# Strassen's seven half-size products for gate and value of the first MoE stage, on chunks of 512 tokens

## What is computed

```python
def _attn_ref(q, k, v, g_norm):            # 4 batches, 8 heads, 576 tokens, head size 64
    kv = np.einsum('bhsd,bhse->bhde', k, v)
    out = np.einsum('bhsd,bhde->bhse', q, kv)
    rms = np.sqrt(np.mean(out * out, axis=-1, keepdims=True) + 1e-06)
    return out / rms * g_norm
def _moe_ref(x, w_gate, w_val, w_out):     # 512 -> 1536 -> 512
    g = x @ w_gate
    silu = g * (1.0 / (1.0 + np.exp(-g)))
    return silu * (x @ w_val) @ w_out
def _moe2_ref(x, w_in, w_out):             # 512 -> 2048 -> 512
    h = x @ w_in
    return (np.maximum(h, 0.0) + np.log1p(np.exp(-np.abs(h)))) @ w_out
```

## Time and profile before

| | us |
|---|---|
| median of 3 runs | 936.55 (936.08 to 937.48) |
| profiled execution | 937.88 |
| its span | 936.03 |
| last product of the first stage issued, from the span's start | 514.2 |
| TensorE busy in the span | 906.2 |
| VectorE busy | 540.1 |
| ScalarE busy | 342.0 |
| GpSimd busy | 91.1 |

### The profile page before, as it was taken

How to read it: one execution, slowest core, us unless ns; L and a number is a source line. 1 busy time by engine, 2 the same in 40 slices (tenths; PEclk the granted TensorE clock), 3 DMA queues, 4 the chain that set the end, 5 groups by cost and what they waited for, 6 DMA issues and landing times.

```text
span 936.0 us, 13451 instructions
## 1 busy us (share of the span) xinstructions
PE 906.2 (97%) x5128; PEld 856.7 (92%) x5128; DVE 540.1 (58%) x1006; ACT 342.0 (37%) x597; POOL 91.1 (10%) x43
## 2 busy tenths in 40 slices
PE   6899899999999999999999699999999999999998
PEld 5789899999999999999999589999998999999997
DVE  3643344453444224224344997887877878878875
ACT  1435413232241001000222344545545554554543
POOL 2424400000000000000243900000000000000000
PEclk9999999999999999999999799999999999999999
DMA  9954461153111000000022300000000000000000
GB/s 251 164 155 125 134 133 26 42 114 73 44 45 56 1 1 1 0 0 0 26 88 91 113 1 1 34 0 0 34 0 0 34 0 0 34 0 0 34 1 34
DMA packets 84189, 44.18 MB, mean 47 GB/s; under 512 B 40768, under 2 KB 76736, under 8 KB 84160
## 3 DMA queue, kind: packets, MB, share of 16 engines
q1 hardware_dynamic: 84000, 43.80, 18.0%
q10 hardware_dynamic: 160, 0.00, 0.0%
HBM read 35.52 MB, written 8.26 MB: 47 GB/s over the span
## 4 chain that ended last, share of the span: by engine, by line
PE 87%; DVE 4%; DMA 3%; SPq 2%; ACT 2%; issue 1%; POOL 0%; DVEq 0%
PE bank L534 21%; PE bank L535 21%; PE bank L536 21%; PE bank L589 7%; PE bank L590 7%; PE bank L588 7%; DMA stage<-in_moe_w_out 2%; PE bank L460 2%; PE bank L475 1%; DMA v_rest<-in_v 1%; SPq L305 1%; ACT arena L664 1%; DVE x_lo L850 1%; DVE g_hi L872 0%; ACT L651 0%
## 5 line engine op out<-in xcount | busy, mean ns | idle before, releaser
L534 PE MATMUL bank<-x_hi,arena 128*128 128x384 f32 x960 | 324.8, 338 | 9.0 <-DVE x_lo L850 5.5
L536 PE MATMUL bank<-x_hi,arena 128*128 128x384 f32 x960 | 323.0, 336 | 0.0
L535 PE MATMUL bank<-x_lo,arena 128*128 128x384 f32 x960 | 322.6, 336 | 0.0
L534 PEld LDWEIGHTS bank<-x_hi,arena 128*128 128x128 f32 x960 | 180.9, 188 | 16.1 <-DVE x_lo L850 6.6
L535 PEld LDWEIGHTS bank<-x_lo,arena 128*128 128x128 f32 x960 | 181.0, 189 | 3.8
L536 PEld LDWEIGHTS bank<-x_hi,arena 128*128 128x128 f32 x960 | 181.1, 189 | 0.0
L881 DVE TENSOR_TENSOR act_a<-act_a,bank 128x384 f32<-128x384 f32 x72 | 39.8, 553 | 228.2 <-PE bank L536 227.0
L686 ACT ACTIVATE act_a<-bank 128x384 f32<-128x384 f32 x72 | 35.4, 492 | 289.6 <-PE bank L536 289.6
L422 POOL TENSOR_TENSOR arena<-stage,arena 128x1024 fp32r<-128x1024 f32 (+1 forms) x28 | 80.8, 2886 | 432.0 <-ACT arena L671 380.7
L707 ACT ACTIVATE act_a<-bank 128x384 f32<-128x384 f32 x96 | 47.3, 493 | 192.2 <-PE bank L536 192.2
L590 PE MATMUL bank<-arena,g_lo 128*128 128x512 f32 x288 | 113.8, 395 | 0.0
(11 more groups left out here) (55 smaller groups left out, 807.4 us busy)
## 6 DMA issues: line engine op xcount, KB each, us to landing
stage<-in_moe_w_out SPq DMA_DIRECT2D x28, 256.0 KB, 4.2
out_dram<-out_stage SPq DMA_DIRECT2D x18, 256.0 KB, 2.1
...
```

The costliest lines, as they stand in the source:

```text
L534: nc.tensor.matmul(ps, hi, rhs_hi, start=first, stop=False)
L535: nc.tensor.matmul(ps, hi, rhs_lo, start=False, stop=False)
L536: return nc.tensor.matmul(ps, lo, rhs_hi, start=False, stop=last)
```

## The change

**Seven products.** The four products of gate and value with two halves of the contraction (256 features each) and two halves of a chunk (256 tokens each) form a 2x2 by 2x2 block product. It is done with Strassen's seven products in Winograd's form instead of eight. A chunk has now `CH1` = 512 tokens; there are `NC1` = 4 such chunks, so `SEVEN` = 48 steps, and 12 further steps (`up_plain`) for the last 256 tokens, with gate and value as before. One product is 2 tiles of the contraction by 3 passes, 6 matmuls of 256 columns; `up_seven` has 7 of them, which go round banks 0 to 3 (`ps_of`). `down1` has 12 matmuls of 512 columns.

**Sums after the products.** VectorE adds up the banks: two additions in `add_early`, five in `add_late`, each of 256 columns with one input in a bank and one in SBUF; ScalarE copies the first product to `p1`. Gate and value stand in `s_buf` and `val`, one buffer each; silu, the product with the value, the rounding (now on ScalarE, `hi_g`) and the low part (`lo_g`) are done there for 512 columns.

**Sums ahead of the products, of the weights.** The split weights no longer fit. `raw1` keeps all 12 raw slices, loaded once, and each step splits them anew for the step after next: four sums of 256 columns on VectorE (`weight_sums`, into the one buffer `s_sum`), the rounding on ScalarE (`hi_raw` 768 columns, `hi_s` 1024, `hi_down` 512), the low parts on GpSimd (`lo_raw` 768, `lo_s` 1024, `lo_down` 512), into `w_up` and `w_down`, two buffers each.

**Of x.** For each chunk four sums of 512 columns on GpSimd (`x_sums`, at step 10), seven operands rounded on ScalarE (`hi_x`), and 14 low parts of 256 columns on VectorE (`lo_x`, at step 11). `s_buf` has only one buffer, so `add_early` waits for `lo_g` of the step before (`g_split`).

**Attention.** k'v runs in steps 0 and 1, tiles at `TILE_AT` = (2, 4, 6, 7, 9), both behind `down1` and in the bank of the seventh product. ScalarE copies a tile to SBUF first (`keep_o`) and squares it there; `normalize_kept` multiplies in SBUF. VectorE and ScalarE do a tile's work in the step after it.

**Second stage.** The same work. The first 8 slices of its weights are split by ScalarE and VectorE (`split_low2`) in the 12 plain steps, the last 8 by GpSimd alone after the last product of the first stage. `split_x` of its first chunk stands three steps ahead of the end of the first stage.

```diff
 def _(pool):
+        def lo_raw(k):
+            pool.wait_ge(hi_raw_ready, k)
...
+            nc.gpsimd.tensor_tensor(w_up[k % 2][:, 1, 0:size], src, w_up[k % 2][:, 0, 0:size].bitcast(F32),
+                                    ALU.subtract).then_inc(w_raw_ready, 1)
...
+        for k in range(STEPS1):
+            if k:
+                lo_down(k)
+            if k % NF1 == NF1 - 2 and k // NF1 + 1 < NC1:
+                x_sums(k // NF1 + 1)
+            if k + 2 < STEPS1:
+                lo_raw(k + 2)
+            if k + 2 < SEVEN:
+                lo_s(k + 2)
...
 def _(pe):
+            for t in range(2):
+                a, b = slice(op * QUAD + t * P, op * QUAD + (t + 1) * P), slice(t * HALF, (t + 1) * HALF)
+                last = passes(ps_of(k, x)[:, 0:HALF], w[:, 0, a], w[:, 1, a], xc[:, slot, 0, b], xc[:, slot, 1, b],
+                              t == 0, t == 1)
+            last.then_inc(prod_done, 1)
...
+            product(k, S3, 3)
+            pe.wait_ge(p1_kept, k + 1)
+            product(k, A22, 4)
+            pe.wait_ge(c11_ready, k + 1)
+            product(k, S1, 5)
+            pe.wait_ge(u2_ready, k + 1)
+            product(k, S4, 6)
...
+        for k in range(1, SEVEN):
+            up_seven(k)
+            down1(k - 1)
+            if k // NF1 < NATT:
+                attention_slot(k // NF1, k % NF1)
...
 def _(act):
+            keep_p1(k)
+            if tile:
+                square_kept(c + 1, TILE_AT.index(f - 1))
+            if k:
+                hi_down(k)
...
+            hi_raw(k + 2)
+            silu(k)
...
+            if k + 2 < SEVEN:
+                hi_s(k + 2)
+            hi_g(k)
...
 def _(dve):
+        def weight_sums(k):
...
+            dve.wait_ge(w_s_ready, k)
+            n = 4 * (k - 1)
+            nc.vector.tensor_tensor(s_sum[:, 0, :], a21, a22, ALU.add).then_inc(s_ready, 1)
+            nc.vector.tensor_tensor(s_sum[:, 2, :], a11, a21, ALU.subtract).then_inc(s_ready, 1)
+            dve.wait_ge(s_ready, n + 2)
+            nc.vector.tensor_tensor(s_sum[:, 1, :], s_sum[:, 0, :], a11, ALU.subtract).then_inc(s_ready, 1)
+            dve.wait_ge(s_ready, n + 3)
+            nc.vector.tensor_tensor(s_sum[:, 3, :], a12, s_sum[:, 1, :], ALU.subtract).then_inc(s_ready, 1)
...
+            dve.wait_ge(g_split, k)
+            dve.wait_ge(p1_kept, k + 1)
+            dve.wait_ge(prod_done, done_before(k) + 2)
+            nc.vector.tensor_tensor(s_buf[:, 0:HALF], p1[:, :], ps_of(k, 1)[:, 0:HALF], ALU.add).then_inc(c11_ready, 1)
...
+            add_late(k)
...
+                weight_sums(k + 2)
+            glu(k)
```

More of the change, by code:

```diff
@@ L40 @@
 ROWS = [P] * J + [REST]
+BLK = 32
+BB = S // BLK
+NA = P // BLK
+NATT = B - 1
+HALF = 256
+CH1 = 2 * HALF
+NC1 = TOKENS // CH1
+CB1, HB = CH1 // BLK, HALF // BLK
+SEVEN = NC1 * NF1
+STEPS1 = SEVEN + NF1
+OPS = 7
+A11, A12, A22, S1, S2, S3, S4 = range(7)
+XSLOTS = 10
+QUAD = 2 * P
+RAW1 = 4 * QUAD + DM
+UP1 = OPS * QUAD
+KV_AT = (0, 1)
+TILE_AT = (2, 4, 6, 7, 9)
+X_NEEDED = [4, NT + 4, 2 * NT + 3, 3 * NT + 3, 4 * NT]
 CH = 384
@@ L558, in down1 @@
+        def down1(k):
+            c, f = divmod(k, NF1)
+            n = width(k)
+            pe.wait_ge(w_down_ready, k + 1)
+            pe.wait_ge(g_split, k + 1)
             if f == 0:
                 pe.wait_ge(acc_free, c + 1)
+            w = w_down[k % 2]
             for t in range(KT):
[L561 to L562 removed]
+                a = slice(t * P, (t + 1) * P)
+                last = passes(acc_ps[t][:, 0:n], w[:, 0, a], w[:, 1, a], g_hi[k % 2][:, 0:n], g_lo[k % 2][:, 0:n],
+                              f == 0, f == NF1 - 1)
@@ new lines, in _ @@
+        store_x(NT - 2, xt_ps0[(NT - 2) % 2])
+        for j in range(1, 4):
+            hi_x(0, j)
+        hi_raw(1)
+        for j in range(4, OPS):
+            hi_x(0, j)
+        hi_s(1)
+        keep_p1(0)
+        store_x(NT - 1, xt_ps0[(NT - 1) % 2])
+        hi_raw(2)
+        silu(0)
+        hi_s(2)
+        hi_g(0)
+        for k in range(1, SEVEN):
+            step(k)
+        for k in range(SEVEN, STEPS1):
+            f = k - SEVEN
+            if f == 1:
+                store_y(NC1 - 1)
+            hi_down(k)
+            silu_plain(k)
+            if k + 2 < STEPS1:
+                hi_raw(k + 2)
+            hi_g(k)
+            for n in range(DVE_LOW2):
+                if step_under(n) + 1 == k:
+                    split_high2(n)
@@ L829, in normalize, with lo_x @@
                                     ALU.mult).then_inc(xn_ready, 1)
-        def split_x(n, chunk, used=None, count=0, tiles=range(KT), scaled=True):
-            for t in tiles:
+        def lo_x(c, j):
+            dve.wait_ge(xc_hi_ready, OPS * c + j + 1)
+            for t in range(2):
+                last = nc.vector.scalar_tensor_tensor(
+                    xc_part(c, j, 1)[:, :, t, :], x_operand(c, j)[:, :, t, :], gain[:, 0:1],
+                    xc_part(c, j, 0)[:, :, t, :].bitcast(F32), ALU.mult, ALU.subtract)
+            last.then_inc(xc_ready, 1)
@@ L836, in split_x @@
+        def split_x(n, chunk, used=None, count=0):
+            for t in range(KT):
                 if used is not None and t < KT - 1:
@@ new lines, in _ @@
+        dve.wait_ge(t_ready, 1)
+        nc.vector.tensor_tensor(x_sum(0, 1), x_block(0, 1, 1), x_sum(0, 0), ALU.subtract).then_inc(t_ready, 1)
+        dve.wait_ge(t_ready, 2)
+        nc.vector.tensor_tensor(x_block(0, 0, 1), x_block(0, 1, 1), x_block(0, 0, 1), ALU.subtract).then_inc(t_ready, 1)
+        lo_x(0, 1)
+        nc.vector.tensor_tensor(x_sum(0, 2), x_sum(0, 1), x_block(0, 1, 0), ALU.subtract).then_inc(t_ready, 1)
+        lo_x(0, 2)
+        lo_x(0, 3)
+        weight_sums(1)
+        for j in range(4, OPS):
+            lo_x(0, j)
@@ L886, in softplus @@
+        for k in range(SEVEN):
+            step(k)
+        for k in range(SEVEN, STEPS1):
+            lo_g(k - 1)
+            glu_plain(k)
+            for n in range(DVE_LOW2):
+                if step_under(n) + 1 == k:
+                    split_low2(n)
+            if k == STEPS1 - 3:
+                dve.wait_ge(acc_free, 2)
+                split_x(0, bass.ds(0, CB))
+        lo_g(STEPS1 - 1)
         def softplus(c, f):
```

872 lines of the change are left out of this document (528 added, 344 removed).

## The result

The kernel with the seven products takes 1070.72 us (median of 4 runs, 1070.28 to 1071.20), the one before on the same chip 937.01 (median of 4, 936.08 to 938.40). The ratio is 1.1426, with a 95% interval from 1.1406 to 1.1445: 134 us slower. The profiled execution has a span of 1069.4 us.

What follows compares the result with a forecast made beforehand. VectorE and GpSimd taking turns on SBUF reads, not TensorE, would bound the first stage: 46 + 508 + 4 + 30 + 31 + 5 + 60 + 21 + 421.8 = 1126.8 us of span, so 1127 us; range 1005 to 1190.

Steps and rivals of the forecast that it cites:

- 47 steps at the plain step's length: First stage, seven-product steps: VectorE and GpSimd taking turns, additions behind lo_g; 10.8 us each, 508 us.
- what attention, chunk ends and clock add to them: Additions to the 47 steps: turns 4, tiles 30, x_sums and lo_x 31, fill_pairs 5, half clock 21 us.
- twelve plain steps of 256 tokens: Last 12 first-stage steps, without seven products: 5.1 us of excluding VectorE and GpSimd work each, 60 us.
- The rival with slow matmuls: First-stage products: a 256-column matmul takes up to 0.172 us, 30 us more in all, 1157 us; 3 in 100.
- the walk: Seven-product step followed instruction by instruction through all engines until it repeats; next E at 10.8 us.
- E: In each seven-product step, the moment TensorE has issued the seventh product; predicted to recur every 10.8 us.
- the clock: Sixth and seventh product at half clock after long TensorE gaps, nine tile steps and six around chunk ends: 1.4 us each, 21 us.
- the tile step: Step with an attention tile: extra VectorE work lets GpSimd slip ahead of lo_g; 0.9 to 3.2 us, 2.0 taken, 15 tiles 30 us.
- a turn: In 12 steps, turns at L1039 and L1045 make add_late later, mostly behind lo_raw; 0.35 us each, 4 us.
- the rival with half clock everywhere: Gaps before the sixth product halve TensorE's clock in the other 32 steps too, 1.4 us each; 1172 us, 22 in 100.
- the second rival: Seven-product steps: turns, but only the amount of excluding work counts, 8.8 us a step; 991 us, up to 1080; 15 in 100.
- TensorE sets the pace: First stage: engines don't exclude each other, TensorE's 7.70 us decides the step; 920 us, 10 in 100.

Runs made afterwards that it cites:

- e1: Changed kernel with GpSimd's low-part subtractions of the weights in steps 1 to 47 replaced by memsets of about the same length; one run, 951.51 us.
- e2: Changed kernel with GpSimd's low-part subtractions of the weights cut to 32 columns from step 4 on; one run, 956.50 us.
- e3: Changed kernel, complete, with ScalarE's rounding of g moved ahead of its rounding of the weight sums; 1031.82 us, ratio 1.1015 to the kernel before.
- e10: Follow-up with low parts moved to VectorE and reordered, plus plain steps alternating s_buf halves and L1157 behind lo_g; 979.92 us, 13.9 less than without the plain-step edits.

## Why the prediction was right, and where it was off

The sign, the mechanism and the range held; the loss was forecast at 190 us and measured at 134. The time was 56 us too high, 57 by its span. By its own sum, in us of span (a step's end is again the moment when TensorE has issued the seventh product):

| term | predicted | measured |
|---|---|---|
| start to the first step's end | 46 | 48.8 |
| 47 steps at the plain step's length | 508 (10.8 each) | 471 (10.03 each) |
| what attention, chunk ends and clock add to them | 91 | 58 |
| twelve plain steps of 256 tokens | 60 | 72.4 |
| rest | 421.8 | 419.4 |
| span | 1126.8 | 1069.4 |

Two terms were 70 us too high together, two others 15 too low and the rest 2 too high; a part of the miss is hidden by the opposite ones.

**The bound.** From the earlier trace rows the prediction read that VectorE and GpSimd take turns, and from the earlier trace rows which instructions don't exclude each other. Both held, instruction by instruction, and e1 and e2 show that this is the cost: without it the same program has steps of 7.78 us. One reading of the earlier trace rows was off, without consequence: GpSimd's copy starts 0.47 us, not 0.3, ahead of the end of VectorE's instruction. The 1.04 us estimated for its own length holds; in e1 such a copy (L511) takes 1037 ns.

**TensorE's work.** Predicted were 0.118 us for a matmul of 256 columns and 7.70 for a step. The timeline of TensorE in after has them:

```profile
575.67 0.28 PE L609 MATMUL bank<-xc,w_up 128*128 128x256 f32 x1
575.79 0.28 PE L607 MATMUL bank<-xc,w_up 128*128 128x256 f32 x1
```

They start 0.12 us apart, and e1's step of 7.78 is 0.08 over the 7.70. The rival with slow matmuls falls. The formula of the Trainium skill (TensorE: Matmul & The Clock Gate, Back-to-back issue gap) gave 0.109 us, which the trace exceeds by a tenth.

**The plain step, 37 us of the 57.** The step of the walk that failed is the one that let a single weight sum in ahead of `lo_raw`. The second sum starts at 509.30 and L460 at 509.41, so two sums are through at their usual length; only the third takes the turn, and the sums end at E + 3.9, not 4.44. I had the right engines and turns, and was wrong by a tenth of a microsecond on who comes first. That is 0.57 of the 0.77 us by which the step is shorter. The other 0.2 are small change behind it: GpSimd starts 0.08 us after ScalarE's end, not 0.14, L466 takes 2.38 us for 2.44, and L1150 ends 0.56 behind it, not 0.63. The order of all later parts of the walk was as written: L1150 near 2.7 us (2.46 here), `lo_s` ahead of it, `add_early` right behind, a wait of TensorE for L1108 of about 2 us (1.70).

**Attention, chunk ends, clock: 33 us of the 57.** In each of the first three chunks the first two steps (with k'v) take 3.1 us more than plain ones together, the next eight 6.5 in sum, the last two 9.5 to 10.2; three times, 58. Predicted were 39 for the chunk ends with their share of the clock, and 52 for the rest. The ends measure 29, tiles, turns and k'v also 29. Of these terms the tile step was mis-sized most: the eight steps between are each 0.5 to 1.2 us over a plain one, or 1.3 for each of the five tiles if all is put down to them, where I took 2.0 for the tile, 0.35 for a turn and 1.4 for the clock. Its lower bound of 0.9 was the nearer end. Which of the small instructions slips in where was not followed up.

**The clock.** I had put 21 us on it. Granted clock (last but two) by stretch, in after:

```profile
112.40:115.20 2.80, 2.64 (x13) 2.64 (x14) 2.54 (x7) 0.00 (x0) 0.79 (x1) 0.57 0.56 172
145.20:147.00 1.80, 1.67 (x13) 1.67 (x14) 1.76 (x6) 0.00 (x0) 0.76 (x1) 1.00 0.00 0
161.00:178.00 17.00, 11.22 (x64) 10.38 (x63) 16.65 (x25) 8.48 (x14) 10.01 (x6) 0.80 0.07 16
178.00:190.00 12.00, 6.15 (x33) 5.55 (x33) 10.97 (x21) 3.15 (x6) 3.85 (x2) 0.77 0.00 1
510.00:520.00 10.00, 8.27 (x56) 7.37 (x55) 8.75 (x14) 3.74 (x6) 6.05 (x4) 1.00 0.00 0
```

The plain steps, with a wait of TensorE of 1.7 us in each, keep 1.00; that refutes the rival with half clock everywhere, to which I had given 22 in 100. The first two rows are the sixth and seventh product of two tile steps, each behind a wait of 1.87 us for L1108: in one the clock is at 1.2 GHz (0.57 on average), in the other at 2.4. Nine tile steps (the fifth, seventh and tenth of each of the first three chunks) have such a wait (1.87 to 1.89 us), and in seven of them the clock falls for some or all of the two products. It falls too around a chunk's end (0.80 and 0.77 on average over such stretches), and the first step's last two products run at half clock (0.21 us a matmul), behind a wait of 3.30 us for L1108; that is 1.3 of the 2.8 us that the start was too low. In a plain step the two products take 1.54 us. They take 1.0 to 1.2 us more in nine of steps 1 to 47 (three tile steps and the two around each chunk's end) and 0.2 to 0.4 more in four tile steps, about 11 us in all (an estimate, added up from the starts of the matmuls). So the price of 1.4 us was somewhat high, and of the fifteen steps for which it was reckoned nine paid in full. How much of the 58 us this is can't be said: the step at 285 us, with 0.17 us more in the two products, takes 10.86 us, its counterparts at full clock 10.65 and 10.67.

**Better packed?** The measured 1070 lies in the band that I had given to the second rival, 991 to 1080. Its mechanism was `lo_g` getting in ahead of `lo_s`, and that did not happen: L466 starts first in 43 of the 48 steps, and in the other five the two don't meet. What packed better was the weight sums. The forecast's chain stands, with one weight sum fewer behind the turn; but both rival and forecast allowed this number, so it is the order of L466 and L1150 that decides between them. And e3, where `lo_g` does get in first, gives 1032, not 991: the chain counts as well as the amount.

**TensorE sets the pace.** That rival was priced at 920 for a kernel in which nothing excludes anything. e1 is nearly that kernel and takes 951.5, so the price was too low. It left out the twelve steps of 256 tokens, in which GpSimd still reads in e1 too (72.3 us, not 12 x 4.25 = 51), and the chunk ends, which stay 8.1 us over two plain steps (GpSimd's `x_sums` still read there). Together that is 45 us, more than the missing 31.5; it wasn't accounted for further.

**Plain steps, 12 us too low.** I had added up excluding work (5.1 us a step). Six of the eleven intervals between the starts of `silu` (L866) are 6.4 to 6.6 us, and one is 7.9. Timeline of after:

```profile
606.26 0.38 ACT L866 ACTIVATE s_buf<-bank 128x256 f32<-128x256 f32 x1 [3.30 <-DVE g_lo L1150]
...
607.67 2.41 POOL L460 TENSOR_TENSOR w_up<-raw,w_up 128x1024 fp32r<-128x1024 f32 x1 [1.78 <-ACT w_up L821]
608.88 2.28 DVE L1157 TENSOR_TENSOR arena<-stage,arena 128x1024 fp32r<-128x1024 f32 x1 [1.78 <-ACT arena L895]
...
611.09 1.48 DVE L1150 TENSOR_TENSOR g_lo<-s_buf,g_hi 128x256 fp32r<-128x256 f32 x1
```

`lo_g` stands behind L1157, that behind GpSimd's subtraction, and `silu` of the next step behind `lo_g`: a chain, which the sum of amounts doesn't see. e10 cuts it, and takes 14 us off the whole.

**The rest** of the kernel, 421.8 predicted, 419.4 measured: nothing to add.
